# Attention and two expert networks on one core: the first expert block routed from the first batch alone

## The reference

```python
# attention: B, H, S, D = 2, 8, 768, 64; block, window = 32, 16
k_sum = k.reshape(B, H, nb, block, D).max(axis=3)
v_sum = v.reshape(B, H, nb, block, D).mean(axis=3)
mask_l = np.abs(pos[:, None] - pos[None, :]) < window
scores_all = concatenate([where(mask_l, scale * q @ k.T, -1e9), scale * q @ k_sum.T + log(block)])
a = softmax(scores_all);  x = a @ concatenate([v, v_sum])     # x: 1536 tokens of 512
# 8 experts, each token to one: w1 [8, 512, 1024], w2 [8, 1024, 512]
logits = x @ w_gate;  e = argmax(logits);  gate_w = softmax(logits)[e]
out[mask_e] = gate_w * (maximum(x[mask_e] @ w1[e], 0) @ w2[e])
# second network: w_in [512, 2048], w_out [2048, 512]
h = out @ w_in;  result = maximum(0.01 * h, h) @ w_out
```

## Time and profile before

| | |
|---|---|
| median of 3 runs | 567.29 us (566.76 to 570.0) |
| the profiled execution | 572.47 us, its span 570.7 us |
| PE busy | 529.0 us (93%) |
| DVE, ACT, POOL busy | 281.6, 255.3, 71.9 us |
| mean granted TensorE clock | 0.958 |
| attention, until the last value matmul | 98.24 us |
| first expert matmul | 127.75 us |
| first matmul of the second network | 300.41 us |

### The profile page before, as it was taken

The page is one execution under the profiler, slowest core; times in us unless marked ns, Lnnn a source line. Parts: engine busy times, 40 slices in busy tenths (PEclk is TensorE's granted clock), DMA queues, the critical chain, the costliest instruction groups (busy, mean ns, idle before and its releaser), DMA issues.

```text
span 570.7 us, 9187 instructions
## 1 busy us (share of the span) xinstructions
PE 529.0 (93%) x3152; PEld 433.3 (76%) x3153; DVE 281.6 (49%) x535; ACT 255.3 (45%) x539; POOL 71.9 (13%) x108
## 2 busy tenths in 40 slices
PE   4799998169999999899979999999999999999997
PEld 3377777158888889788867888888888888888885
DVE  3568775635523444754205723754642663642631
ACT  4468776224433434653304633631643550553520
POOL 6314510232014013120200000000000000000000
PEclk9979999568999999989998999999999999999999
DMA  9999641259047046561352063053164041330001
GB/s 211 225 207 227 162 117 51 62 195 350 25 162 239 19 174 216 197 221 36 148 176 83 3 218 148 1 185 121 63 221 147 0 165 61 142 147 0 0 18 55
DMA packets 75386, 74.16 MB, mean 130 GB/s; under 512 B 45408, under 2 KB 47456, under 8 KB 75360
## 3 DMA queue, kind: packets, MB, share of 16 engines
q1 hardware_dynamic: 71072, 62.28, 36.4%
q0 software_dynamic: 2560, 8.39, 4.6%
q10 hardware_dynamic: 1728, 3.15, 1.6%
HBM read 63.32 MB, written 10.49 MB: 129 GB/s over the span
## 4 chain that ended last, share of the span: by engine, by line
PE 84%; SPq 4%; ACT 3%; DMA 3%; issue 3%; DVE 2%; POOL 1%; POOLq 0%; ACTq 0%; DVEq 0%
PE psum L1173 13%; PE psum L1174 12%; PE psum L1175 12%; PE psum L1189 12%; PE psum L1187 12%; PE psum L1188 12%; PE psum L1055 2%; PE psum L1088 2%; ACT p_sb L594 2%; PE psum L1071 2%; PE psum L1142 1%; PE psum L1046 1%; SPq L309 1%; PE psum L1030 1%; DMA k_nat<-in_k 1%
## 5 line engine op out<-in xcount | busy, mean ns | idle before, releaser
L1173 PE MATMUL psum<-xT_hi,w_hi 128*128 128x512 f32 (+1 forms) x320 | 124.0, 388 | 4.1 <-DVE w_lo L902 2.3
L1174 PE MATMUL psum<-xT_lo,w_hi 128*128 128x512 f32 (+1 forms) x320 | 123.5, 386 | 0.0
L1175 PE MATMUL psum<-xT_hi,w_lo 128*128 128x512 f32 (+1 forms) x320 | 123.1, 385 | 0.0
L1187 PE MATMUL psum<-w_hi,h_hi 128*128 128x512 f32 x296 | 115.9, 392 | 0.0
L1189 PE MATMUL psum<-w_hi,h_lo 128*128 128x512 f32 x296 | 115.2, 389 | 0.0
L1188 PE MATMUL psum<-w_lo,h_hi 128*128 128x512 f32 x296 | 115.2, 389 | 0.0
L902 DVE TENSOR_TENSOR w_lo<-w_raw,w_hi 128x512 fp32r<-128x512 f32 x80 | 51.4, 686 | 60.7 <-ACT w_hi L651 60.5
L1173 PEld LDWEIGHTS psum<-xT_hi,w_hi 128*128 128x128 f32 x320 | 61.6, 193 | 16.8 <-DVE xT_lo L912 5.0
L1175 PEld LDWEIGHTS psum<-xT_hi,w_lo 128*128 128x128 f32 x320 | 61.6, 193 | 11.9
L1174 PEld LDWEIGHTS psum<-xT_lo,w_hi 128*128 128x128 f32 x320 | 61.7, 193 | 11.6
L671 ACT ACTIVATE h_small<-psum 128x512 f32<-128x512 f32 x48 | 28.7, 598 | 89.9 <-PE psum L1175 89.9
(11 more groups left out here) (134 smaller groups left out, 530.7 us busy)
## 6 DMA issues: line engine op xcount, KB each, us to landing
w_raw<-in_moe_w_in SPq DMA_DIRECT2D x12, 1024.0 KB
w_raw<-in_moe_w_out SPq DMA_DIRECT2D x6, 2048.0 KB, 8.3
w_raw<-in_moe_w SPq DMA_DIRECT2D x8, 1024.0 KB
w_raw<-in_moe_w SPq DMA_DIRECT2D x4, 2048.0 KB, 8.9
vw<-in_v SPq DMA_DIRECT2D x20, 192.0 KB, 4.9
k_nat<-in_k SPq DMA_DIRECT2D x12, 256.0 KB, 5.1
q_nat<-in_q SPq DMA_DIRECT2D x12, 256.0 KB, 5.1
x_rows<-x_cur ACTq DMA_DIRECT2D x12, 256.0 KB, 3.8
```

The source lines that it names most:

```text
L1173: mm(h, w1_hi[:, c, cols], xT_hi[:, c, 0:n], start=(c == 0), stop=False)
L1174: mm(h, w1_hi[:, c, cols], xT_lo[:, c, 0:n], start=False, stop=False)
L1175: last = mm(h, w1_lo[:, c, cols], xT_hi[:, c, 0:n], start=False, stop=(c == KD - 1))
L1187: mm(y_ps[s % 2], h_hi[:, c, rows], w2_hi[:, c, :], start=(c == 0), stop=False)
```

## The change

The first expert block no longer waits for the routing of all tokens.

- In units 14 to 21 (batch 1's attention) DVE, PE and POOL route the first batch: `choose(0)`, `rank_first`, `first_expert` (the expert with most tokens of batch 0), `first_slots`, `first_hots`, and an inversion of 12 small matmuls. Up to 384 tokens (`SUB0` = 3 tiles) of that expert are block 0. SP loads that expert's w1 and w2 behind unit 16, POOL gathers the three tiles, ACT and DVE do five of the eight w1 splits in units 19 to 23, and PE transposes the rows around unit 23's values.
- Block 0 runs straight-line with 384 columns. Inside it stand the last tile's logits, `choose(1)`, counts, places, the second inversion and tables for all tokens that are left, and the gather and transposes of block 1. The counting is done by matmuls (`total_ps`, `place_ps`, `ends_ps`) instead of DVE's running sums; the two one-hot products (rows and tiles parts) are accumulated in one column each instead of being added by DVE.
- The loops over blocks begin at 1; `MAXB` is 11 (10 before). Tokens of the first expert beyond its 384 slots go into later blocks with the second batch's.
- Batch 1's key pieces go to units 2 to 9 (`K_STEP` = 2), the mean of batch 1 to unit 10 (`MEAN_STEP`; unit 10 before, too). The v rows are loaded one step earlier. POOL builds the routing constants before it spreads batch 1's means. The second batch's queries reuse the first batch's buffer.
- SBUF is laid out by hand, so that w1, the rows and their high part overlie batch 0's keys and values, and w2 and the hidden activations batch 1's.
- PE's fill of 10 matmuls ahead of block 0 and ACT's zeroing of six PSUM banks are gone.

```diff
-K_STEP = 1
-V_STEP = K_STEP + PIECES
+K_STEP = 2
+MEAN_STEP = K_STEP + PIECES
+ROUTE_STEP = 14
+W1_STEP = UNITS - 5
+W1_LEFT = UNITS - W1_STEP
...
-MAXB = TOK // ROWS + E - 1
+REST = TOK - S // E
+MAXB = 1 + (REST + E * (ROWS - 1)) // ROWS
...
 sync:
-                if t == 4:
+                if t == 3:
                     load_v_rows()
...
+            sp.wait_ge(experts_ready, 1)
+            sp.wait_ge(o_done, B_UNITS)
+            first_e = sp.value_load(first_plan[0:1, 0:1], min_val=0, max_val=E - 1)
+            load_w1(first_e)
+            sp.wait_ge(kt_transposed, B * PIECES)
+            sp.wait_ge(vsum_done, B)
+            load_w2(first_e)
...
 gpsimd:
+            pool.wait_ge(past_ready, 1)
+            then(tt(is_tile[:, tiles, 0:SUB0], past[:, :, 0:SUB0], past[:, :, 1:SUB], ALU.subtract))
+            for i in range(2):
+                tt(hot_tile[:, tiles, i, 0:SUB0], is_tile[:, tiles, 0:SUB0],
+                   tok_part[:, i, tiles].unsqueeze(2).to_broadcast([P, QT, SUB0]), ALU.mult).then_inc(hot_tile_ready, 1)
...
+            pool.wait_ge(tokens_ready, 1)
+            gather(token_of_slot, x_dram[0:S, :], SUB0)
+            pool.wait_ge(tiles_ready, 1)
+            for i in range(2):
+                tt(hot_tile[:, :, i, :], is_tile[:], tok_left[:, i, :].unsqueeze(2).to_broadcast([P, T, LATER_TILES]),
+                   ALU.mult).then_inc(hot_tile_ready, 1)
...
+            pool.wait_ge(tokens_ready, 2)
+            pool.wait_ge(rows_transposed, KD)
+            gather(token_of_slot[:, SUB:2 * SUB], x_dram[:, :], SUB)
...
 scalar:
+                if n >= W1_STEP:
+                    split_w1(0, n - W1_STEP)
+            split_rows(0, 0, KD, xt_first_ps, ROWS0)
...
+            for f in range(KF):
+                relu_hidden(0, f, ROWS0)
+                if f == 0:
+                    copy_xT(T - 1)
+                split_w2(0, f)
+                if W1_LEFT + f < KF:
+                    split_w1(0, W1_LEFT + f)
+                if f == 5:
+                    gate_exp()
+            second_product(0, 1, True, y_sb, None, 0, 2)
+            for i in range(4, 8):
+                split_w1(1, i)
+            split_rows(1, 0, KD)
+            second_product(0, None, True, y_sb, None, 2, SUB0)
...
 vector, in the loop over units:
+                if n == ROUTE_STEP:
+                    choose(0)
+                if n == ROUTE_STEP + 2:
+                    first_expert()
+                if n == ROUTE_STEP + 3:
+                    first_slots()
+                if n == ROUTE_STEP + 4:
+                    first_hots()
+                if n == ROUTE_STEP + 6:
+                    dve.wait_ge(route_step, step[0])
+                    keep_tokens(0, SUB0)
+                if n == ROUTE_STEP + 7:
+                    keep_homes(0, SUB0)
+                if n >= W1_STEP:
+                    split_w1(0, n - W1_STEP)
...
+            for f in range(KF):
+                rest_of_relu(0, f, ROWS0)
+                split_w2(0, f)
+                if W1_LEFT + f < KF:
+                    split_w1(0, W1_LEFT + f)
+                if f == 1:
+                    keep_logits(T - 1)
+                    dve.wait_ge(left_ready, 1)
+                    choose(1)
+                    shift_logits()
+                if f == 3:
+                    count_blocks()
+                if f == 5:
+                    later_experts()
+                    later_slots()
+                if f == 6:
+                    slot_parts(T)
+                    hot_tiles(T, LATER_TILES)
+            hot_rows(T)
+            keep_gates()
+            later_tables()
+            for i in range(8):
+                split_w1(1, i)
+            split_rows(1, 0, KD)
...
 tensor:
+                if n == UNITS - 1:
+                    transpose_first(0, 2)
                 weighted_v(n)
+            transpose_first(2, KD)
...
+            hidden(0, 0, 0, ROWS0)
+            transpose_x(T - 1)
+            hidden(0, 0, 1, ROWS0)
+            gate_logits(T - 1)
+            hidden(0, 0, 2, ROWS0)
+            pe.wait_ge(logits_ready, T)
+            hidden(0, 0, 3, ROWS0)
+            pe.wait_ge(chosen_ready, 2)
+            for t in range(T):
+                last = mm(total_ps, chosen[:, t, :], ones[:], start=(t == 0), stop=(t == T - 1))
+            last.then_inc(totals_done, 1)
+            hidden(0, 0, 4, ROWS0)
+            pe.wait_ge(blocks_ready, 1)
...
+            for f in range(5, KF):
+                hidden(0, 0, f, ROWS0)
+            second_part(0, 0, 0, KF // 2)
+            pe.wait_ge(hot_row_ready, 2)
+            pe.wait_ge(hot_tile_ready, 4)
+            invert(inv_ps, T, LATER_TILES)
+            second_part(0, 0, KF // 2, KF)
+            second_product(0, 1, 2)
+            transpose_rows(1, rows_gathered, 2, 0, 2)
+            second_part(0, 2, 0, KF // 2)
+            transpose_rows(1, rows_gathered, 2, 2, KD)
+            second_part(0, 2, KF // 2, KF)
...
-            with pe.Fori(0, MAXB) as j:
+            with pe.Fori(1, MAXB) as j:
```

More of the change, by code:

```diff
@@ L554, in _ @@
+            pool.wait_ge(experts_ready, 2)
+            n_blocks = pool.value_load(plan[0:1, MAXB:MAXB + 1], min_val=2, max_val=MAXB)
+            pool.wait_ge(homes_ready, 2)
+            with pool.Fori(1, MAXB) as j:
                 with pool.If(j < n_blocks):
```

927 lines of the change are left out of this document (523 added, 404 removed).

## The result

| | us |
|---|---|
| before, beside it | 568.49 (566.76 to 570.0, 4 runs) |
| after | 580.9 (576.04 to 582.39, 4 runs) |
| ratio | 1.0209, 95% interval 1.0155 to 1.0262 |
| forecast | 562.6, range 555.5 to 570.5 |

The account below looks back on a forecast made before the run. The prediction took TensorE as the bound, with one serial routing gap from 99 to 128 us to win. Second block at 147.4 against break-even 152.1 gave -4.7, off the median 567.29: 562.6 us, range 555.5 to 570.5.

Parts of the forecast that it names:

- T1: Start of the second expert block's first matmul: forecast at 147.4 us, with break-even against the kernel before at 152.1.
- the tail of 130.6: From the second block's start to PE's last expert matmul: two full blocks of 45.3, one-tile blocks of 21.35 and 18.6 us.
- forecast change of -4.7: Whole kernel: second block's start at 147.4 against break-even at 152.1, so 4.7 us faster; bounds -14 to +8.
- Early attention, -4.5: First attention units: moving batch 1's first key piece to unit 2 removes a wait and clock dip, saving 4.5 us.
- Late attention, +3.1, +0.65, +1.6: Units 14 to 23: added routing work +3.1, transposing first rows before unit 23's values +0.65, waiting for those rows +1.6.
- First block, 44.0+1.0: First expert block: 39.0 us of PE work plus waits and reading the plan make 44.0, plus 1.0 for a clock fall.
- The 3.35 ahead of the block: Before the first expert block: 2.05 us waiting for row splits and the last normalising, plus 1.3 for a clock fall.
- Tail and handover: Second block to last expert matmul 130.6 us; then handover to the second network longer by 5.0, ending on a one-tile block.
- rival 2, the wash: Whole kernel: early gain of 4.5 doesn't appear, or first-block routing is that much longer; 567.1 us, chance 0.23.
- Rival 3: Late attention: weights and gathered rows share the DMA, rows land late, price 6 to 8; 568.6 to 570.6 us, chance 0.13.
- Rival 4, the clock: PE's clock falls at four more waits or stays low twice as long, 1.7 us each; 569.4 us, chance 0.07.

Follow-up runs that it names:

- e12: e4's kernel run again, unchanged, on another chip: 570.03 us, ratio 0.9987 to the kernel before.
- e4: Changed kernel with only its expert tiles moved, so every operand starts at 1568 modulo 2048 bytes as before: 567.06 us, ratio 0.9964.
- e13: Kernel before with unused tiles, so w1, xT, w2 and h start where the changed kernel has them modulo 2048 bytes: 579.91 us, ratio 1.0181.
- e3: Changed kernel with its regions moved so all expert operands start at 32 modulo 128 bytes, but differ modulo 2048: 578.79 us, ratio 1.0146.
- e7: Changed kernel with expert tiles placed as in e4 and the load of v_rows one tile later: 567.75 us, ratio 1.0012.
- e11: Changed kernel, expert tiles placed as in e4, VectorE's table building earlier, first expert's w2 requested only after the first block's rows are gathered: 568.47 us, ratio 0.9978.
- e1: Kernel before with one unused 64-byte tile ahead of all attention and expert tiles, shifting them alike: 568.91 us, ratio 0.9982.
- e9: TensorE alone, neither kernel: 50 groups of 96 first-product matmuls differing only in operand starts; 21.90 us when alike modulo 256 bytes, otherwise 0.2 to 0.7 more.

## Why the prediction was wrong, step by step

| mark, us | before | forecast | after | e12 (placed, clock kept) |
|---|---|---|---|---|
| unit 10 begins | 58.9 | 54.4 | 59.0 | 54.8 |
| last value matmul of the attention ends | 98.24 | 99.1 | 103.9 | 97.3 |
| first expert matmul | 127.75 | 102.5 | 105.1 | 98.9 |
| second block, T1 | - | 147.4 | 153.65 | 147.13 |
| end of the last expert matmul, from T1 | - | 130.6 | 133.1 | 130.9 |
| from there to the second network | 12.67 | 17.7 | 16.4 | 16.7 |
| second network | 270.3 | 270.3 | 277.4 | 268.6 |

- **The step that failed is one the prediction didn't spell out.** "A full block lasts 221.13-175.82 = 45.3 us, so its 192 matmuls are 0.227 apart" was carried over to the changed kernel, in the tail of 130.6 and, silently, in a second network of unchanged length. The edit moved every tile of the experts; the diff shows the new `region` allocator, and I priced none of it. The runs showed 0.2333 instead. By e4 and e12 against the result this is 580.9-567.1 = 13.8 us, by e13 9.9, and by count (1656 matmuls of 512 columns, 6.6 ns each) 10.9; it is the sign of the result. No rival had it.
- **The profiled execution.** Its span is 580.6, and the forecast change of -4.7 from 570.7 would have made it 566.0. Of the 14.6 between, 6.3 are there at T1, 2.5 come in the tail, 7.1 in the second network, and the handover gives back 1.3. The tail's and the second network's parts are mostly placement; most of the 6.3 is not, as the next points show.
- **Early attention, -4.5.** Right where nothing interferes: no wait for the key load, no clock dip at 28, -4.1 in e12. In the profiled execution the late start (2.4 against the kernel before at unit 1) and the break at 42 us with the clock behind it took all of it back. Over ten profiles of the changed kernel and its variants unit 10 begins at 54.7 to 60.4 (median 56.9); in six of the kernel before and its variants, at 57.1 to 59.5 (median 59.0). That is a gain of about 2 in the median. Counted from unit 1 on it is 4.4: 30.3 us in six of the ten profiles and 34.7 in the kernel before. So the forecast was right for the work, and wrong in taking one start for all. Neither the late start nor the break is in a row that I read.
- **Late attention, +3.1, +0.65, +1.6.** The terms of the +3.1 add up to 3.3. The rows came in time: PE's wait for them, the 1.6, didn't occur. From unit 10 to the last values it took 42.5 us in e12, 3.2 more than the 39.3 before, for 5.35 forecast. The waits behind DVE's and ACT's splits came in every profile with this order (0.66 to 0.68 and 1.57). In the changed kernel, e3 and e7 the clock fell behind them, which cost 2.1 to 3.7 us; in e4 and e12 it didn't. The end was 97.3 in e12 and 103.9 in the profiled execution.
- **First block, 44.0+1.0.** From the first hidden matmul to T1 48.5 in the changed kernel and 48.2 in e12: 3.2 to 3.5 too little. The terms: 384 columns are 0.173 apart in e12, as interpolated, where one hidden tile follows the next (2.08 for twelve), but twelve behind other matmuls take 2.2, which makes 17.2 where the sum had 16.5 (+0.7); the reading of the plan 2.5, not 1.0 (+1.5); rows 1.9, not 1.3 (+0.6). The inversion's wait was 2.84 against 2.7, though behind hot_row, not behind hot_tile. The 3.35 ahead of the block was 1.2 to 1.6, and the attention ended 1.8 sooner than forecast in e12. So T1 came out right there by luck: 1.8 and 1.8 too much against 3.2 too little.
- **Tail and handover.** Five first products, two narrow, as forecast; 130.9 against 130.6, and a handover of +4.0 against +5.0 in e12. The 130.9 is luck in part too: the slow start of 1.5 us came in the second block and not in the last, and the last one waited 1.87 for xT_lo, which the sum hadn't. The second network's 268.6 in e12 is 1.7 less than before because its first product began at the full clock; in e4, the same kernel, it didn't.
- **Rivals.** With placement taken out the outcome is near rival 2, the wash: 0.4% faster by the medians, not clear of the noise. Rival 3 needed rows later than 103 us; PE waited for the first block's rows in no profile, and e11 shows no price of the shared DMA. Rival 4, the clock, was right in kind: two falls behind stalls of PE decide some 2 to 4 us each in the changed kernel and its variants. The kernel before has the like: from unit 1 to unit 10 31.6 us in e1 and 34.7 in the profile.
- **The reference point.** I took the difference against one profiled execution, 5.2 above the median of its kernel. e12's profile is one of the shortest of 19. Set beside the shortest run of the kernel before in each of the four jobs (564.45 to 565.4), 565.05 is no gain; only the medians show the 2.4.

## What to carry to other kernels

When an edit moves tiles, put the starts of all operands of one chain of wide matmuls at the same place modulo 256 bytes, and compare the distance of untouched matmuls before anything else: 22.39 against 21.76 per 96 said more than any wait in the page. A short stall of TensorE can cost 2 to 4 us more than its own length when the clock falls behind it, and it doesn't fall each time; eight throwaway matmuls in a wait of 1.1 to 3 us were worth 3.5 us in the one job that compared them. Removing the wait named last in a chain of table building moves most of it to the next link (2.8 before the inversion became 1.6 more before the rows).

## What the hardware showed that I had not expected

- fp32r matmuls of 128x128 by 512 columns take 0.9 to 3.2% longer when their operands don't start alike modulo 256 bytes of the partition (e9: 21.90 against 22.10 to 22.60 per 96), at a granted clock of 1.00. A single line of the timeline prints 0.39 or 0.40 either way; the mean duration goes from 389 to 392 ns to between 392 and 397. A common shift costs nothing, and at 256 columns there is no price (11.39 before, 11.19 after from first to last start).
- PE can break off inside a group of matmuls for 0.7 to 1.0 us with no semaphore to wait for, at the same instruction in two kernels that differ only in their addresses (42.43 in the changed kernel, 42.21 in e4), and not in other executions of the same code (e12).
- One kernel's executions spread over 6.8 us (e4 and e12, 19 runs: 565.01 to 571.80), and their order largely follows the mean granted clock (0.984 to 0.994 below 567.2 us, 0.976 to 0.985 above 569).
